# A recurrent attention and expert-layer kernel: constants, one weight part, fill-in matmuls and the last group's chunks are moved

## The reference, cut to what matters

```python
# stage 1: B=2, H=8, S=768, D=40
for t in range(S):
    m_new = max(f_gate[t] + m, i_gate[t])
    f_stab, i_stab = exp(f_gate[t] + m - m_new), exp(i_gate[t] - m_new)
    C = f_stab * C + i_stab * outer(v[t], k[t]);  n = f_stab * n + i_stab * k[t]
    y[t] = sigmoid(o_gate[t]) * (C @ q[t]) / max(abs(n . q[t]), 1)
# stage 2: x is (1536, 320), E=4 experts of 1024 hidden columns
out = sum_e p[:, e] * (relu(x @ w1[e]) @ w2[e])
# stage 3: 1536 hidden columns
return ((out @ w_a) * (out @ w_b)) @ w_out
```

## Time and profile before

| what | value |
|---|---|
| median of 3 executions (lowest to highest) | 606.54 us (606.18 to 622.47) |
| the profiled execution's own time | 606.54 us |
| its span, first to last instruction | 604.5 us |
| PE, PEld busy | 597.0, 581.0 us |
| DVE, ACT, POOL busy | 360.0, 293.7, 179.2 us |
| bytes moved | 38.38 MB, mean 63 GB/s |

### The profile page before, as it was taken

The page is one execution under the profiler, slowest core; times in us unless marked ns, Lnnn a source line. Parts: engine busy times, 40 slices in busy tenths (PEclk is TensorE's granted clock), DMA queues, the critical chain, the costliest instruction groups (busy, mean ns, idle before and its releaser), DMA issues.

```text
span 604.5 us, 10937 instructions
## 1 busy us (share of the span) xinstructions
PE 597.0 (99%) x3991; PEld 581.0 (96%) x3991; DVE 360.0 (60%) x705; ACT 293.7 (49%) x622; POOL 179.2 (30%) x246
## 2 busy tenths in 40 slices
PE   7999999999999999999999999999999999999997
PEld 6888899999999999999999999999999999999997
DVE  7877984454474443644544635389796665666555
ACT  5888745424443344433344434656744543444332
POOL 3466430014340134200425101515035521553000
PEclk9999999999999999999999999999999999999999
DMA  4675541003311011410032100212102310120011
GB/s 128 200 227 183 166 127 51 11 1 69 97 40 62 1 47 23 137 40 23 0 71 87 57 12 1 47 25 87 57 12 47 108 58 12 42 51 1 1 67 65
DMA packets 21028, 38.38 MB, mean 63 GB/s; under 512 B 3520, under 2 KB 11280, under 8 KB 20976
## 3 DMA queue, kind: packets, MB, share of 16 engines
q1 hardware_dynamic: 19040, 35.02, 20.0%
q10 hardware_dynamic: 1936, 2.67, 1.3%
HBM read 26.42 MB, written 1.97 MB: 47 GB/s over the span
## 4 chain that ended last, share of the span: by engine, by line
PE 94%; DVE 4%; issue 1%; DMA 1%; ACT 0%; DVEq 0%
PE PS L1697 38%; PE PS L1616 12%; PE PS L1619 12%; PE PS L1617 12%; PE PS L1618 12%; PE PS L1559 3%; PE PS L1528 1%; PE PS L1516 1%; PE PS L1476 1%; PE PS L1502 1%; PE PS L1478 1%; PE PS L1542 1%; DMA dec_r<-llo 1%; DVE pt L1067 0%; DVE acc L1274 0%
## 5 line engine op out<-in xcount | busy, mean ns | idle before, releaser
L1697 PE MATMUL PS<-w2h,hh 128*128 128x320 f32 x528 | 164.9, 312 | 0.0
L1697 PE MATMUL PS<-w2l,hh 128*128 128x320 f32 x528 | 163.4, 310 | 0.0
L1697 PE MATMUL PS<-w2h,hl 128*128 128x320 f32 x528 | 163.2, 309 | 0.0
L1616 PE MATMUL PS<-xop,wop 128*128 128x384 f32 x400 | 138.5, 346 | 0.0
L1619 PE MATMUL PS<-xop,wop 96*128 96x384 f32 x400 | 135.0, 337 | 0.0
L1617 PE MATMUL PS<-xop,wop 128*128 128x384 f32 x400 | 134.8, 337 | 0.0
L1618 PE MATMUL PS<-xop,wop 128*128 128x384 f32 x400 | 134.6, 337 | 0.0
L734 ACT ACTIVATE hh<-c_s 128x384 fp32r<-128x384 f32 x120 | 62.8, 524 | 100.1 <-DVE c_s L1247 27.9
L1697 PEld LDWEIGHTS PS<-w2h,hh 128*128 128x128 f32 x528 | 99.5, 189 | 0.3 <-DVE hl L1224 0.2
L1697 PEld LDWEIGHTS PS<-w2l,hh 128*128 128x128 f32 x528 | 99.7, 189 | 0.0
L1697 PEld LDWEIGHTS PS<-w2h,hl 128*128 128x128 f32 x528 | 99.4, 188 | 0.0
(11 more groups left out here) (146 smaller groups left out, 803.5 us busy)
## 6 DMA issues: line engine op xcount, KB each, us to landing
s<-in_wt SPq DMA_DIRECT2D x24, 256.0 KB, 3.1
kvo<-in_tok SPq DMA_DIRECT2D x12, 480.0 KB, 4.2
wop<-t1h SPq DMA_DIRECT2D x48, 112.0 KB, 2.2
qk<-in_qk_t SPq DMA_DIRECT2D x24, 160.0 KB
s<-in_w SPq DMA_DIRECT2D x12, 320.0 KB, 2.9
wop<-t1l SPq DMA_DIRECT2D x24, 112.0 KB, 2.2
s<-in_w_out SPq DMA_DIRECT2D x12, 160.0 KB, 2.2
out_y<-acc SPq DMA_DIRECT2D x12, 160.0 KB, 1.9
```

The source lines that it names most:

```text
L1616: nc.tensor.matmul(to, ws[0], xs[0], start=opens, stop=False, skip_group_check=True)
L1697: got = nc.tensor.matmul(bank, left, (w2l if part == 1 else w2h)[p][:, f, :], start=opens and part == 0, stop=closes and part == 2)
```

## The change

It does four things. At the start, POOL makes `mask` and `identb` right after `ones` and without the wait for `rows_ready`, then `dec_l`, then `vx` and `state`, and it clears `qk[1]` as its last constant, which DVE no longer does; SP issues the load of `qk[1]` behind the first high rows, and waits for that clearing. PE has one `keep_busy` matmul less ahead of `log_weights(0)`. In group 0 a new function `keep_fed` puts one matmul in each of the slots 0, 1 and 2, with a wait that the bank it writes is free. Weight part 19 is cut one group later (high and low part and sums in group 33, high and low part of the sums in 34). And the second-layer matmuls of the last group are spread otherwise over its seven slots.

```diff
--- before.py
+++ after.py
@@ -219,7 +219,7 @@
 
             return (i // NP1 - 1) * 2 * NP1 + NP1 + i % NP1
 
-        PARTED = {E * NP1 + 2: FIRST, E * NP1 + 3: FIRST}
+        PARTED = {E * NP1 + 2: FIRST, E * NP1 + 3: FIRST + 1}
 
         def a_at(i):
 
@@ -299,7 +299,7 @@
             if turning(n) is not None:
                 return (3, 6, 0, 1, 2, 5, 1, 6, 6, 6) if n <= FIRST else (0, 2, 0, 1, 1, 2, 0, 6, 6, 0)
             if n == NG - 1:
-                return (0, 2, 0, 1, 5, 0, 10)
+                return (0, 2, 1, 1, 3, 3, 8)
             return (4, 5, 5, 5, 8, 5, 4) if n <= FIRST else (0, 3, 2, 2, 5, 4, 2)
 
         def out_bank(u):
@@ -405,10 +405,10 @@
             load_qk(0)
             sp.dma_start(gate_r[:, :, :], late).then_inc(late_in, 16)
             load_kvo(0)
-            sp.wait_ge(qk_zero, 2)
-            load_qk(1)
             load_first_high_row(0)
             load_first_high_row(1)
+            sp.wait_ge(pool_const, 11)
+            load_qk(1)
             sp.wait_ge(m_ready, 1)
             sp.dma_start(m_r[:, 1, :], m[:, P + 1:S + 1]).then_inc(m_in, 16)
             load_kvo(1)
@@ -456,21 +456,21 @@
             nc.gpsimd.tensor_tensor(pick[:, :], identf[0:64, 0:BH], identf[0:64, 32:32 + BH], ALU.add).then_inc(pool_const, 1)
             pool.wait_ge(pool_const, 3)
             nc.gpsimd.memset(ones[:, :], 1.0).then_inc(pool_const, 1)
-            nc.gpsimd.memset(f32(dec_l[:, :, :]), 1.0).then_inc(pool_const, 1)
-            pool.wait_ge(pool_const, 5)
-
-            nc.gpsimd.affine_select(out=dec_l[:, :, :], in_=dec_l[:, :, :], compare_op=ALU.is_ge, fill=0.0, base=PICKED - 1,
-                                    pattern=[[0, NC], [1, P]], channel_multiplier=-1).then_inc(pool_const, 1)
-            pool.wait_ge(rows_ready, 1)
             nc.gpsimd.memset(mask[:, :, :], 0.0).then_inc(mask_ready, 1)
             pool.wait_ge(mask_ready, 1)
 
             nc.gpsimd.affine_select(out=mask[:, :, :], in_=mask[:, :, :], compare_op=ALU.is_ge, fill=NEG, base=STEPS,
                                     pattern=[[0, NP], [1, P - STEPS]], channel_multiplier=-1).then_inc(mask_ready, 1)
             nc.gpsimd.tensor_copy(identb[:, :], identf[:, :]).then_inc(mask_ready, 1)
+            nc.gpsimd.memset(f32(dec_l[:, :, :]), 1.0).then_inc(pool_const, 1)
+            pool.wait_ge(pool_const, 5)
+
+            nc.gpsimd.affine_select(out=dec_l[:, :, :], in_=dec_l[:, :, :], compare_op=ALU.is_ge, fill=0.0, base=PICKED - 1,
+                                    pattern=[[0, NC], [1, P]], channel_multiplier=-1).then_inc(pool_const, 1)
             for b in range(B):
                 nc.gpsimd.memset(vx[b][:, :, D:D1], 1.0).then_inc(pool_const, 1)
                 nc.gpsimd.memset(state[b][:, :, :, :], 0.0).then_inc(pool_const, 1)
+            nc.gpsimd.memset(qk[1][:, :, :, :], 0.0).then_inc(pool_const, 1)
 
             def update_keys(u):
                 c, b = u // B, u % B
@@ -836,6 +836,12 @@
                 if n % (2 * NP1) == 5 and st + 1 < NS:
                     tails_high_s(st + 1)
 
+            def prepare_parted_sums(n):
+
+                for i in PARTED:
+                    if s_at(i) == n:
+                        high_s(i)
+
             def prepare_parted(n):
 
                 for i in PARTED:
@@ -978,14 +984,12 @@
                 keep_u2(n)
                 replicate_late(b1, 2)
                 replicate_late(b2, 5)
-                if b1 is not None:
-                    high_s(E * NP1 + 2)
+                prepare_parted_sums(n)
                 keep_w(n)
                 keep_turn(n, 1)
                 keep_turn(n, 2)
                 high_product(n, 0)
-                if b1 is not None:
-                    high_s(E * NP1 + 3)
+                prepare_parted(n)
                 replicate_late(b1, 3)
                 if b1 is not None:
                     x_high(b1, 0)
@@ -1121,7 +1125,6 @@
 
             nc.vector.memset(m[:, 0:1], NEG).then_inc(dve_const, 1)
             nc.vector.memset(qk[0][:, :, :, :], 0.0).then_inc(qk_zero, 1)
-            nc.vector.memset(qk[1][:, :, :, :], 0.0).then_inc(qk_zero, 1)
 
             def logs_of(i_, f_, before, after, lf, lsum, li, lhi, llo, done, n, first):
 
@@ -1484,6 +1487,15 @@
                 for _ in range(n):
                     nc.tensor.matmul(PS[:, INTER, BUSY_COLS:BUSY_COLS + P], ones[:, :], ones[:, :], start=True, stop=True)
 
+            def keep_fed(n, bank):
+
+                if bank == UPD:
+                    pe.wait_ge(state_ready, 2 * OLD)
+                else:
+                    pe.wait_ge(num_ready, NU - 1)
+                for _ in range(n):
+                    nc.tensor.matmul(PS[:, bank, BUSY_COLS:BUSY_COLS + P], identf[:, :], identf[:, :], start=True, stop=True)
+
             def log_weights(u):
 
                 c, b = u // B, u % B
@@ -1703,7 +1715,10 @@
 
                 if n == 0:
                     if slot == 0:
+                        keep_fed(1, UPD)
                         outputs(NU - 1)
+                    else:
+                        keep_fed((1, 1, 0)[slot - 1], OUT)
                     return
                 if n == 1 and slot == 0:
                     pe.wait_ge(p_ready, 2 * NU)
@@ -1730,7 +1745,7 @@
 
             keep_busy(13)
             products(0)
-            keep_busy(3)
+            keep_busy(2)
             log_weights(0)
             turn_first_logs()
             log_weights(1)
```

## The result

The changed kernel takes 613.7 us in the median of 15 executions (608.77 to 618.8), the kernel before 607.56 us in 15 (605.95 to 622.47). The ratio is 1.0079 with a 95% interval of 1.0052 to 1.0105: slower, by less than 2%, and outside the range of the prediction (605.8 to 609.0). The profiled execution of the changed kernel took 609.79 us, with a span of 607.9. So there are two things to explain: 3.4 us between the two profiled spans, and that the medians are 6.1 us apart. (The ratios leave out executions over 1.5% above the fastest of their kernel, such as three of the changed kernel at 618.4 to 618.8 us; the medians and counts here hold all.)

The account below looks back on a forecast made before the run. The prediction took PE to bound the kernel, busy for 597.0 of 604.5 us. It summed start 0.1, group 0 0.4, weight part 0.1 and last group 0.6 to 1.2, so 606.54 became 607.7 us, range 605.8 to 609.0.

Parts of the forecast that it names:

- Its sign: Whole kernel: slower, by 1.2 us, from 606.54 to 607.7 us.
- four terms: Start +0.1, group 0 +0.4, weight part +0.1 and last group +0.6 us.
- POOL holds DVE up: Start: POOL's memsets hold DVE's L1133 until 6.6, ending 1.0 us late; rival that POOL holds nothing, chance 0.20.
- Everything arrives between 13.5 and 14.2, against 13.77: Start: m_r and qk[1] land about when DVE's second round of logs began before; cost taken as +0.1 us.
- No change within 0.4: Start: the logs' rows go out 1.0 us later but land at 10.55 to 11.05, against 10.66 before.
- The clock: Rival: a longer PE wait ahead of log_weights(0) lowers the attention stage's clock for 16 to 60 us; 622 or more, chance 0.03.
- The wait becomes no longer than 1.5: Start, argument against the clock rival: PE's wait from 10.14 to past 10.66 grows to at most 1.5 us.
- near 8 us: Start: when PE's clock rises from its lower level, read from the kernel before's first 26 passes taking 5.92 us.
- Group 0: Three added matmuls cost 0.69 us in all, partly hidden by PE's waits; 0.4 taken, bounds 0.1 to 0.7.
- The weight part: Group 34: POOL's moved low_s delays DVE by up to 1.1 us; +0.1 taken, bounds -0.1 and +0.5.
- its own waits take most: Group 34: DVE's waits absorb most of its delay of up to 1.1 us, leaving PE +0.1.
- The last group: Second-layer matmuls ahead of the last product delay it and everything behind by 0.59 us; 0.6 taken, bounds 0.3 to 0.7.

Follow-up runs that it names:

- pool_only: Kernel before with POOL's new order and its clearing of qk[1], qk[1]'s load left where it stood; 607.78 us, ratio 1.0018.
- qk_last: Kernel before with qk[1]'s load moved behind SP's copy of m as well; one execution, no time given; PE waits 2.32 us for qk[1].
- kvo_late: Kernel before with the load of kvo[0] behind the first high rows, qk[1]'s load left ahead of them; 608.52 us, ratio 1.0023.
- start_only: Kernel before with the change's start alone (POOL's order and clearing, SP's order, one fill-in less); 610.63 us, ratio 1.0027.
- sp_only: Kernel before with SP's order alone changed (qk[1]'s load behind the first high rows), DVE still clearing both; 609.94 us, ratio 1.0036.
- chunks_only: Kernel before with the last group's new second-layer spread alone; one execution, last matmul 0.60 us later against the group's first product.
- no_start: Changed kernel with the start of the kernel before; 608.27 us, ratio 1.0025 against the kernel before.
- part_only: Kernel before with weight part 19 alone cut one group later; one execution, loses 0.61 us from group 34 to 37.
- fed_only: Kernel before with group 0's three keep_fed matmuls alone; one execution, 0.30 us later at group 1, 0.08 back by group 2.

## Why the prediction was wrong

Its sign and three of its four terms hold. The size fails at the start.

- **POOL holds DVE up: right.** L1136 took 0.76 us and ended behind POOL's last memset, at 6.50 where 6.7 was written. The rows went out at 8.17 (8.35 written) and the first landed in time for a product at 10.65 (10.55 to 11.05). pool_only shows the half alone at +0.13, where +0.1 was taken for the start; that near is luck, since profiles of one start differ by more.
- **"Everything arrives between 13.5 and 14.2, against 13.77": the step that failed.** The prediction followed the first batch's low row only, and wrote that the rows gain by the load being queued behind them. ACT issues two low rows, 1.6 us apart, and the second went out with the load. It also let `m_r` land in 2.7 us with the load just ahead of it. The landings were 3.34 us for the row, 3.2 and 4.0 for the copies. `m_r` came at 14.8 where 13.65 was written, and DVE's second round at 14.89. "No change within 0.4" was true of the first batch and 1.0 wrong for the second. qk_last and kvo_late show that it is the load, and any load, in that place. With the clock up the start costs 0.7 us, a rough size from one execution of start_only (607.45); in the profiled execution with its short fall it is 1.94.
- **The clock: the rival's mechanism came about, its chance and its size were wrong.** The rival had PE fall back after a longer wait, for 16 to 60 us or not at all, and got 0.03 for it. It fell in 14 of 16 executions, for the attention stage's first microseconds: 3.3 us in the profiled one, 13.7 in those of start_only and sp_only. At half the clock PE's work there costs 1 to 5 us, in the longest more: the changed kernel's executions at a mean of 0.981 take 618.4 to 618.8. Its condition was wrong as well. "The wait becomes no longer than 1.5" looked at one wait; there were two, 1.55 and 1.77 us, with 1.1 us of PE work between them. The prediction took the rise "near 8 us" as fixed; it came sooner in the changed kernel's profile, and in chunks_only's, where it came sooner still, PE waits 1.54 us with the start of the kernel before. And 38 of 91 executions of the kernel before fall too, which one profile with the clock up could not show, but the 622.47 in its three times could have made one ask.
- **Group 0: right.** 0.23 us for 0.4, within its bounds: 0.30 paid and 0.08 given back behind group 1.
- **The weight part: under-sized.** 0.62 us for 0.1, just over the upper bound of 0.5. The collision was foreseen to the row (1.58 for 0.49); "its own waits take most" was the mistake. DVE had 0.45 us of idle time behind it, and lost 1.1.
- **The last group: right.** 0.58 us for 0.6. Product 5 waits 0.40 where 0.3 was written. The idle in front of the tiles is not one of 0.6 but 0.20 and 0.29, together 0.28 more than the 0.21 before: two matmuls fewer stand behind the last product (17 for 19, at 0.147 each), and the other 0.3 is product 5's wait.

With the clock up the sum of the measured terms is 0.7 + 0.2 + 0.6 + 0.6 = 2.1 us, and the medians with the clock up are 608.8 (two executions) and 606.73; that they agree to 0.1 is in part luck, as the first term is one execution. The prediction's 1.2 would have been off by 0.9 there; the rest of the miss is the clock.

What stays open: why the low stretch is short in one execution and four times as long in another with the same start, why kvo_late is deep in one of 10 when start_only and sp_only are in 5 and 6 of 10, and whether the moment of the clock's rise decides.

## What to carry to other kernels

When a bulk load is moved in a queue, list every small transfer that goes out near its new place, on all queues and with the time of its issue, and not only the first; the last of them decides. Where a profile shows PE waiting in its first microseconds, fill those waits with cheap matmuls before anything else is tuned there (here 3 of 34 executions with a fall for 38 of 91, and no gain in the median), and judge a change by many executions, sorted by their mean granted clock: one profile with the clock up says nothing of the median. A cover of 0.45 us does not hide a collision of 1.1 us.

## What the runs showed that I had not expected

- A few fill-ins more in the early waits make falls of the granted clock rare: 3 of 34 executions with waits filled, 38 of 91 with them as they were, though no wait of PE's in these starts was longer than 2.4 us.
- All seven profiles with a fall are ones in which the clock had risen early (the first 26 passes in 5.23 us or less), and of those in which it rose late (5.65 or more) none fell.
- A row of 4 KB issued beside a bulk load took 3.0 to 3.9 us to land; in pool_only, where the load had been issued by 7.05 and the row went out at 8.17, it took 2.62.
- A run of memsets on POOL held a one-input DVE instruction on 16 partitions up to its end (0.76 us for 0.28), while a scan beside a memset took 0.74 and two-input instructions beside memsets 0.41, as without them. The hold need not last to the end of the run: in kvo_late L1167 takes 0.54 us for 0.89 and ends at 9.10, with POOL's last memset running from 9.01 to 9.43.
- The same start differs by up to 0.9 us between profiled executions: `log_weights(0)` begins at 10.91 in the kernel before, at 10.53 in no_start, 10.68 in part_only, 11.16 in fed_only and 10.30 in chunks_only, all five with the same start. Terms of 0.1 us at the start can't be told from that.
